# Attention and two MLP layers: three chunks of 384 tokens instead of two batches of 576, and rotation by pairs of heads

## The reference

```python
B, H, S, D = 2, 8, 576, 64                      # q, k, v
q_rot, k_rot = (rotate(q), rotate(k))           # rotary embedding over positions 0..575
scores = scale * np.matmul(q_rot, k_rot.transpose(0, 1, 3, 2))
attn = np.exp(scores - scores.max(-1, keepdims=True))
attn = attn / (np.sum(attn, axis=-1, keepdims=True) + 1e-09)
x = np.matmul(attn, v)                          # -> x: 1152 tokens x 512 (heads side by side)
h = x @ w_in                                    # 512 -> 2048
x = (h * (1.0 / (1.0 + np.exp(-h)))) @ w_out    # first layer
h = x @ w_in2
y = np.where(h > 0.0, h, np.exp(np.minimum(h, 0.0)) - 1.0) @ w_out2   # second layer
```

## Time and profile before

| | |
|---|---|
| median of 3 runs | 624.61 us (624.39 to 626.56) |
| the profiled execution | 624.31 us |
| its span in the trace | 622.2 us |
| instructions | 12042 |
| mean granted TensorE clock | 0.985 of 2.4 GHz |
| busy: TensorE, VectorE, ScalarE, GpSimd | 563.5, 351.0, 328.0, 329.3 us |
| moved by DMA | 58.45 MB, mean 94 GB/s |

### The profile page before, as it was taken

The page is one execution under the profiler, slowest core; times in us unless marked ns, Lnnn a source line. Parts: engine busy times, 40 slices in busy tenths (PEclk is TensorE's granted clock), DMA queues, the critical chain, the costliest instruction groups (busy, mean ns, idle before and its releaser), DMA issues.

```text
span 622.2 us, 12042 instructions
## 1 busy us (share of the span) xinstructions
PE 563.5 (91%) x4160; PEld 550.0 (88%) x4160; DVE 351.0 (56%) x502; ACT 328.0 (53%) x617; POOL 329.3 (53%) x239
## 2 busy tenths in 40 slices
PE   1776767779999999999989999999999999999997
PEld 1665656669999999999989999999999999999997
DVE  5899999967787643439898643324441003664000
ACT  1586766857676554547666654535553224555220
POOL 4789776227566674638375673323335443335340
PEclk9799998999999999999999999999999999999999
DMA  6442222031322424131412422213223222222310
GB/s 209 173 125 88 87 86 86 22 119 65 128 96 68 155 74 149 51 126 52 155 61 67 155 87 84 74 70 86 84 76 97 83 82 68 85 84 93 113 54 38
DMA packets 27106, 58.45 MB, mean 94 GB/s; under 512 B 3009, under 2 KB 5057, under 8 KB 27073
## 3 DMA queue, kind: packets, MB, share of 16 engines
q1 hardware_dynamic: 25920, 55.65, 28.4%
q10 hardware_dynamic: 1152, 2.36, 1.0%
HBM read 55.64 MB, written 2.36 MB: 93 GB/s over the span
## 4 chain that ended last, share of the span: by engine, by line
PE 64%; DVE 17%; issue 10%; POOL 5%; ACT 2%; DMA 1%; DVEq 0%; ACTq 0%; SPq 0%; POOLq 0%
PE banks L854 54%; DVE neg_max L580 3%; PE banks L844 3%; PE banks L811 2%; POOL w_lo L265 2%; DVE sum_eps L615 2%; DVE act_buf L651 2%; PE banks L802 2%; DVE v_st L596 1%; PE banks L803 1%; DVE pt_lo L603 1%; DVE q_tile L562 1%; DVE g_lo L603 1%; DMA k_raw<-k 1%; PE banks L818 1%
## 5 line engine op out<-in xcount | busy, mean ns | idle before, releaser
L265 POOL TENSOR_TENSOR w_lo<-w_raw,w_hi 128x512 fp32r<-128x512 f32 x128 | 170.3, 1336 | 243.3 <-ACT w_hi L385 243.3
L854 PE MATMUL banks<-x_lo,w_hi 128*128 128x288 f32 x512 | 110.4, 297 | 2.1 <-DVE head_out L626 1.0
L854 PE MATMUL banks<-g_lo,w_hi 128*128 128x288 f32 x512 | 109.8, 296 | 0.0
L854 PE MATMUL banks<-g_hi,w_lo 128*128 128x288 f32 x512 | 109.7, 296 | 0.0
L854 PE MATMUL banks<-x_hi,w_lo 128*128 128x288 f32 x512 | 109.6, 296 | 0.0
L854 PE MATMUL banks<-g_hi,w_hi 128*128 128x288 f32 x512 | 109.5, 296 | 0.0
L854 PE MATMUL banks<-x_hi,w_hi 128*128 128x288 f32 x512 | 109.4, 295 | 0.0
L385 ACT CAST w_hi<-w_raw 128x512 fp32r<-128x512 f32 x128 | 78.7, 615 | 48.5 <-PE banks L854 46.0
L580 DVE TENSOR_REDUCE neg_max<-banks 128x1 f32<-128x576 f32 (+1 forms) x80 | 59.9, 749 | 45.7 <-PE banks L803 45.6
L854 PEld LDWEIGHTS banks<-x_lo,w_hi 128*128 128x128 f32 x512 | 82.3, 189 | 3.4 <-DVE head_out L626 1.2
L854 PEld LDWEIGHTS banks<-g_lo,w_hi 128*128 128x128 f32 x512 | 82.5, 189 | 0.0
(11 more groups left out here) (89 smaller groups left out, 872.9 us busy)
## 6 DMA issues: line engine op xcount, KB each, us to landing
w_raw<-w SPq DMA_DIRECT2D x128, 256.0 KB, 2.7
k_raw<-k SPq DMA_DIRECT2D x15, 576.0 KB, 3.8
q_raw<-q SPq DMA_DIRECT2D x15, 576.0 KB, 4.7
v_raw<-v SPq DMA_DIRECT2D x16, 160.0 KB, 2.3
out<-act_buf ACTq DMA_DIRECT2D x8, 288.0 KB, 2.1
table<-rope SPq DMA_DIRECT2D x2, 288.0 KB, 3.6
k_raw<-k SPq DMA_DIRECT2D x2, 288.0 KB, 3.9
q_raw<-q SPq DMA_DIRECT2D x2, 288.0 KB, 5.0
```

The source lines that it names most:

```text
L265: nc.gpsimd.tensor_tensor(w_st[LO][:, slot, :], w_raw[:, slot, :], w_st[HI][:, slot, :].bitcast(F32), ALU.subtract).then_inc(w_lo_done, 1)
L854: last = nc.tensor.matmul(dst[:, a, :], w_st[wp][:, slot, c * P:(c + 1) * P], src[xp][:, tile * S + a * HALF:tile * S + (a + 1) * HALF], s ...
```

## The change

The 1152 tokens are taken as three chunks of 384 (three full query tiles of 128). The middle chunk holds the last 192 tokens of batch 0 and the first 192 of batch 1. Attention of chunk 0 stands alone, both layers of chunk 0 run beside the attention of chunk 1, both of chunk 1 beside that of chunk 2, and both of chunk 2 alone. The weights are so loaded and split three times (192 units) and not twice. A unit is 4 tiles x 3 products of 384 columns, its result fits one PSUM bank, and three banks take turns. The keys and values of up to ten heads stay in SBUF (`k_st`, `v_st`). In the middle chunk, tile 1 has queries of both batches: its scores are two accumulated pairs of products, with the other batch's columns zero (`PADS`), and the value products are made for each batch on 192 columns.

Rotation takes the two heads of a pair at once, one in each half of the partitions. GpSimd forms `queries_lo` and `values_lo`, VectorE forms `keys_lo` and copies the queries' high part to the other half (`queries_dup`). The row sums are inverted for a pair of heads, with each reciprocal written 64 times (128x384), so that three transposes spread them and `scale_outputs` reads them from PSUM; `copy_row` goes. In a step, ScalarE's order is now `hidden_act`, `probs_hi`, `hidden_hi`, `weight_hi`, `exp_tile`. VectorE's is `hidden_mul`, the attention's operations, `hidden_lo`. All loops are unrolled.

```diff
-QT = 5
-UNITS = FT + KT * (FT // KT)
+CHUNKS, CT, QN = 3, 384, 3
+ITERS = CHUNKS * H
+SLOTS = 10
+UNITS = 64
+ALL_UNITS = CHUNKS * UNITS
...
+        END_BANK, PV_BANK = 2, 3
+        def mlp(use):
+            return banks[:, 5 + (use + 1) % 3, 0:CT]
...
         @block.vector
+            def invert_sums(p):
+                dve.wait_ge(exp_done, 2 * QN * (p + 1))
+                nc.vector.tensor_scalar(sum_eps[:, :, :], row_sum[:, p % 2, :, :], EPS, None, ALU.add) \
+                    .then_inc(eps_done, 1)
+                dve.wait_ge(eps_done, p + 1)
+                if p:
+                    dve.wait_ge(row_done, p)
+                nc.vector.reciprocal(inv_sum[:, :, :, :], sum_eps[:, :, :].unsqueeze(3).broadcast_to([P, QN, 2, D])) \
+                    .then_inc(inv_done, 1)
...
+            def keys_lo(s):
+                rows, others = rows_of[s % 2], other_rows_of[s % 2]
+                dve.wait_ge(k_hi_done, s + 1)
+                nc.vector.scalar_tensor_tensor(k_st[others, s % SLOTS, :], k_raw[s // 2 % 2][rows, 0, :], SCALE,
+                                               k_st[rows, s % SLOTS, :].bitcast(F32), ALU.mult, ALU.subtract) \
+                    .then_inc(k_lo_done, 1)
+
+            def queries_dup(i):
+                dve.wait_ge(q_hi_done, i + 1)
+                nc.vector.tensor_copy(placed(q_one[i % 2], i, other_rows_of[i % 2]),
+                                      placed(q_one[i % 2], i, rows_of[i % 2]).bitcast(F32)).then_inc(q_dup_done, 1)
...
+            for n in range(H * QN):
+                i, t = n // QN, n % QN
+                p = i // 2
+                max_tile(n + 1)
+                if n:
+                    probs_lo(n - 1)
...
+                if t == 0 and i:
+                    end_lo(i - 1)
+                    if i % 2 == 0:
+                        invert_sums(p - 1)
+                    elif p:
+                        scale_outputs(p - 1)
...
+            for n in range(ALL_UNITS):
+                c, i, j = n // UNITS, H + n // 8, n % 8
...
+                evict_a(n - 1)
+                if j == 0 and i <= ITERS:
+                    if beside and n:
+                        max_tile(QN * i)
+                    probs_lo(QN * i - 1)
+                    end_lo(i - 1)
+                    if i % 2 == 0:
+                        invert_sums(p - 1)
+                    if first:
+                        evict_b(n - 1)
+                        add_outputs(i - 1)
+                        scale_outputs(p - 1)
+                        output_lo(p - 1)
+                if beside:
+                    if j == 1 and i % 2 == 0 and i >= H + 2:
+                        if p < 8:
+                            keys_lo(i + 1)
+                        queries_dup(i + 1)
+                    if j == 3:
+                        max_tile(QN * i + 1)
+                        probs_lo(QN * i)
+                        if not first:
+                            add_outputs(i - 1)
...
+                if not (j == 0 and first and i <= ITERS):
+                    evict_b(n - 1)
...
         @block.scalar
...
+                evict_a(n - 1)
+                if j == 0:
+                    probs_hi(QN * i - 1) if i <= ITERS else None
+                    if i <= ITERS:
+                        end_hi(i - 1)
+                if beside and j == 3:
+                    probs_hi(QN * i)
+                if beside and j == 5:
+                    probs_hi(QN * i + 1)
+                evict_b(n - 1)
+                if n + AHEAD < ALL_UNITS:
+                    weight_hi(n + AHEAD)
+                if beside:
+                    if j == 0:
+                        exp_tile(QN * i)
...
         @block.tensor
+            def score_tile(n):
...
+                if c == 1:
+                    parts = (((0, first_head),), ((P, first_head), (2 * P, second_head)), ((3 * P, second_head),))[t]
+                else:
+                    parts = ((t * P, second_head if c == 2 else first_head),)
...
+            def products(src, tile, slot, m, dst, start, stop):
                 for n, (wp, xp) in enumerate(((HI, LO), (HI, HI), (LO, HI))):
+                    last = nc.tensor.matmul(dst, w_st[wp][:, slot, m * P:(m + 1) * P], src[xp][:, tile, :],
+                                            start=start and n == 0, stop=stop and n == 2)
...
+            for c in range(CHUNKS):
+                start, ahead = UNITS * c, H * (c + 1)
+                if c:
+                    transpose_tile(QN * ahead - 1)
+                    if ahead < ITERS:
+                        score_tile(QN * ahead)
+                hidden_unit(start, range(KT - 1))
+                value_products(ahead - 1)
+                spread_sums(ahead // 2 - 1)
+                hidden_unit(start + 1, range(KT - 1))
+                hidden_unit(start + 2, range(KT - 1))
+                for u in range(3):
+                    hidden_unit(start + u, range(KT - 1, KT))
+                for u in range(3, UNITS):
+                    i, j = ahead + u // 8, u % 8
+                    if i < ITERS:
+                        if j == 0:
+                            transpose_tile(QN * i - 1)
+                            score_tile(QN * i)
+                        if j == 2:
+                            value_products(i - 1)
+                        if j == 3:
+                            transpose_tile(QN * i)
+                            score_tile(QN * i + 1)
+                        if j == 5:
+                            transpose_tile(QN * i + 1)
+                            score_tile(QN * i + 2)
+                            if i % 2 == 0 and u >= 8:
+                                spread_sums(i // 2 - 1)
...
```

More of the change, by code:

```diff
@@ L850, in products @@
[L850 removed]
+                    for m, (col, slot) in enumerate(parts):
+                        nc.tensor.matmul(scores(n)[:, a, :], q_one[par][:, col:col + P], k_st[:, slot, keys],
+                                         start=m == 0, stop=False)
+                        last = nc.tensor.matmul(scores(n)[:, a, :], q_two[par][:, col:col + P], k_st[:, slot, keys],
+                                                start=False, stop=m == len(parts) - 1)
```

1308 lines of the change are left out of this document (571 added, 737 removed).

## The result

The changed kernel takes **678.7 us** (median of 4 runs, 676.19 to 679.92) where the kernel before takes 624.5 (4 runs, 623.52 to 626.56): ratio **1.086**, 95% interval 1.082 to 1.090. It is 54 us slower; I had forecast 628 and a range of 602 to 642.

A forecast was written before the change was run, and what follows sets the result against it. TensorE was taken as the bound (busy 91%), with VectorE pacing the exposed attention. 101 + 486.6 + gaps of 5, 15, 10 and 5 + 3.0 gave a 625.6 us span; 2.1 more gave 628 us, range 602 to 642.

The forecast's parts named there:

- Term 1: Exposed attention before the first MLP product, paced by VectorE: 101 us instead of 128.4.
- Six operations of a pair of heads read that way: 3.3: Exposed attention: VectorE operations running against GpSimd cost 0.55 us more each, 3.3 us for a pair of heads.
- The reciprocal: VectorE's inversion of row sums on 128x384: 3.2 us, its excess growing with the elements; 0.6 us if the excess is fixed.
- Rival A: The reciprocal on VectorE is cheap, 0.6 us, so the kernel takes 609 us; chance 0.18.
- Term 2: TensorE's own work from the MLP's start, at 173.5 ns per product of 384 columns: 486.6 us, 9.8 more than before.
- rival C: TensorE's 13.5 ns overhead is per column, so 384 columns cost 178 ns and the kernel takes 636 us; chance 0.17.
- rival D: TensorE's overhead shrinks with fewer, wider products, 162.5 ns each, so the kernel takes 613 us; chance 0.06.
- Term 3: TensorE's gaps behind the MLP's start: 5 last-chunk ELU, 15 ELU beside attention, 10 chunk starts, 5 restarts, in us.
- 0.48 + 0.04 + 0.35 + ... = 2.57 us for an ELU unit: Serial loop of a hidden ELU unit through ScalarE and VectorE: 2.57 us, against 2.08 on TensorE.
- the 5 us of the last chunk and part of the 15 beside attention: Gaps in ELU stages from the loop through ScalarE and VectorE: 5 us in the last chunk alone, 15 beside attention.
- at starts of chunks only (10 us): At the starts of three chunks, value products wait for end_lo and spread_sums for the reciprocal: 10 us of gaps.
- Rival B: Three banks absorb the loops of ScalarE and VectorE, gaps stay at 14 us, so the kernel takes 607 us; chance 0.14.

The follow-up runs named there:

- the form in PSUM: Changed kernel with ELU as min(exp(h) - 1, max(h, 0)), the maximum written in place in PSUM: 662.5 us, ratio 1.065.
- the five edits: Changed kernel with weight_hi before hidden_hi, ELU's maximum in PSUM, reciprocal on 128x6 plus copy, queries_dup on ScalarE, value products one unit later: 596.3 us, ratio 0.955.
- order edit: Changed kernel with ScalarE's weight_hi moved back between hidden_act and hidden_hi: 636.7 us, ratio 1.022.

## Why the prediction was wrong, point by point

- **Term 1, exposed attention: 101 forecast, 114.3 measured. Two steps failed. The first is "I keep VectorE's present cost of running against it ... Six operations of a pair of heads read that way: 3.3".** That is 0.55 us an operation, 13 us in all, taken from the mean of `queries_lo`. Measured are 1.66 more for each of nine `keys_lo` and 1.22 for each of eight `queries_dup`, 24.7 us. A held operation does its own work when GpSimd pauses, and GpSimd's operations come here with hardly a pause between them, so three of the nine `keys_lo` took 4.1 to 4.3 us. A mean of other operations could not give that; the earlier trace rows had the sign of it, the epsilon's 128x5 operation in SBUF with 154 ns at the least and 2878 at the most. Moving `keys_lo` to VectorE and adding the copy put the two operations that are held longest into its list; the experiments that take away the copy or the rotation give 22 to 23 us back at the start. The second is "VectorE was busy 94% of this stretch, so 83.5": its share is 87%. `scale_outputs` waits 2.1 us three times for `spread_sums` (L545 above), which I did not have. By VectorE's account, 87.0 us are busy where my list had 78.5, and 12.5 idle where I had 5.0; that is 16.0 more, less the 2.7 that I had added for the clock, 13.3. The holds beyond my 13 make 11.5 of the 16.0 and the idle time 7.5; the reciprocal gives 2 back.
- **The reciprocal: 3.2 us forecast, 2.55 measured.** That is (2553 - 190) / 379 = 6.2 ns an element in all, where I had 7 to 10 (6 to 9 beside the 1.05), and the time is below the 2.9 I had as bound. The choice against a fixed excess was right. The figure worked out from the Trainium skill, "VectorE: DVE Perf Modes", note on the 8 slices, 3.3 us as eight cycles an element, is 0.8 us above the measurement, which decides. Rival A's price of a cheap reciprocal, 19 us on the total, compares with 13.5 measured for one that costs 0.93 with its copy.
- **Term 2, TensorE's own work: 486.6 forecast, 487.6 measured; right.** 384 columns are 173.3 ns apart, so the 13.5 ns over 2.4 GHz are per product (13.3 here), not per column (rival C, 178), and they do not shrink (rival D, 162.5). A value product of 192 columns is 111 ns from the next, 109 forecast.
- **Term 3, the gaps: 35 forecast, 69 measured. The step that failed is the 0.35 in "0.48 + 0.04 + 0.35 + ... = 2.57 us for an ELU unit".** The same hold that term 1 counted was left out here, where it strikes every unit, since the order makes `weight_lo` start just ahead of L574 each time: 3.23 us a unit. With the form in PSUM the loop takes 2.64 and the stage is 6.7 us over TensorE's own, where I had 5 to 6 for a loop of 2.57; that the two lie so close is in part luck, since the one unit with L574 in SBUF and nothing beside it took 2.46. So the closed loop was right as a mechanism and one term of it was not. I had taken the first part's price from a single unit (0.46 us). Its mean in the kernel before was half as much again:

```profile
L651 DVE TENSOR_SCALAR act_buf<-act_buf 128x576 f32<-128x576 f32 x32 | 21.9, 683 | 7.5 <-ACT act_buf L395 6.9
```

  Beside attention the same error stands in every window's sum ("30.6; odd window 24.9"), with `hidden_lo`, which reads two SBUF tiles, at 0.72 on average instead of 0.55.
- **What the order of ScalarE's list costs was right as a mechanism and too small as a size.** In my sum it was the 5 us of the last chunk and part of the 15 beside attention. Measured it is, with the hold that it brings, 42 us of 54 in the kernel after, and 24 in the kernel before, where nothing else was changed.
- **Value products wait for VectorE: I had this at starts of chunks only (10 us), and it came inside the chunks too.** The waits there are up to 3.8 us long, and the four longest of the seven (3.6 to 3.8 us) cost more than their length, since products at the lower clock follow them. Two windows of the kernel after, the wait that ends at 246.2 and what follows it:

```profile
242.00:246.00 4.00, 0.65 (x4) 0.32 (x2) 3.90 (x7) 2.65 (x7) 1.20 (x2) 1.00 0.20 74
246.00:250.00 4.00, 3.79 (x20) 3.82 (x21) 3.24 (x5) 1.77 (x6) 2.05 (x3) 0.62 0.20 72
```

```profile
246.60 0.27 PE L756 MATMUL banks<-pt_hi,v_st 128*128 128x192 f32 x1
246.71 0.28 PE L756 MATMUL banks<-pt_lo,v_st 128*128 128x192 f32 x1
...
247.78 0.41 PE L756 MATMUL banks<-pt_hi,v_st 128*128 128x192 f32 x1
248.00 0.41 PE L756 MATMUL banks<-pt_lo,v_st 128*128 128x192 f32 x1
```

  The value products start at their usual distance of 0.11 us, and from 0.7 us on stand 0.22 apart: the granted clock is 0.62 in this stretch, at the lower of its levels (1.2 GHz) for most of it, behind 3.57 us in which TensorE did nothing. In the first stretch, with TensorE idle almost half of it, it is 0.77 on average (0.93 before).
- **Rival B (loops absorbed, gaps of 14 us, 607) is the kernel that the edits make.** With the loop opened and less of VectorE's work held, the gaps are 16.6 us and the time is 596. The chunks of 384 are not what makes the changed kernel slower than the one before: the order, the ELU form, the copy of the queries on VectorE, the long reciprocal and the place of the value products are, in the sum of the five edits. `keys_lo` stayed on VectorE in all of them; what giving it back to GpSimd would bring was not measured.

What is left open. The ELU stage of chunk 0 is at 55 to 58 us in all kernels made from the one after that keep `queries_dup` on VectorE or have no order edit, and falls only with both (50.8); in it TensorE waits for `pt_lo` 3.6 us (3.3 with the order edit) and for `x_lo` 2.7. I can say that VectorE's list is late there, and which operations are in it, not how much each one costs. And the edits do not add up alone and together, so a price of one edit holds only for its neighbours.

## What to carry to other kernels

Price a VectorE operation that touches only SBUF with what GpSimd has in flight when it is released, in every loop, not as a mean: if the release of both comes from the same list of ScalarE a fixed time apart, they meet nearly every time (15 of 16 units here). Where an engine's list has one operation that nobody is waiting for soon (here `weight_hi`, needed three units later), put it where the engine would wait anyway; at the end of a loop that goes through two engines it is added to each turn. And when a wait is removed, look for the second one that ended just before it: moving `weight_lo` forward gained 4.4 us and lost 4.8, while 23 us lay with another engine.

## What the runs showed of the hardware that I had not expected

- Whether GpSimd holds a VectorE operation goes by its operands in every row here. With SBUF alone: TENSOR_SCALAR 128x384 0.35 us or 1.17, CAST 64x384 0.35 or 1.57 on average, SCALAR_TENSOR_TENSOR 64x576 0.75 or up to 4.31. With one operand in PSUM: L572 (the tanh layer's step, 128x384) takes 0.54 to 0.56 us in all 48 cases, and in 39 of them GpSimd works for at least half of its time. A TENSOR_SCALAR of the same shape in place in PSUM takes 0.57 next to a running `weight_lo`. The Trainium skill, "SBUF — State Buffer", "Who interferes with whom", says just this: copies, casts and scalar operations from SBUF in a two-port mode, and operations with two SBUF inputs, exclude GpSimd's, and the one that starts first blocks the other whole. The traces agree, in both directions. VectorE's side is above. GpSimd's: of the 192 `weight_lo` in the kernel after, 171 start with no VectorE operation in SBUF alone under way and take 1.27 to 1.30 us; the other 21 take 1.28 to 1.81, 1.56 in the median. The rule spoke against this change, and my forecast did not use it.
- The hold can outlast the operation that causes it: L557 waited through three GpSimd operations in a row, until there was a pause of 0.08 us between two of them.
- Taking 12.6 us of copies off VectorE brought the first product 23 us forward, because the `keys_lo` left in its list met GpSimd less often (seven of nine at 0.75 us, none of nine in the kernel after). How long such a list takes hangs on when its operations fall, and not on their number alone.
